# A mixture-of-experts kernel whose second layer changes its operands: split fp32r matrices stream, results are turned afterwards

## The chip, the cores and the metric

The kernel runs on one core of one Trainium2 chip. The metric is the device time of one execution in microseconds; a kernel's time is the median of several runs.

## The reference

Three stages in a row on 768 tokens with 512 features, cut to what matters:

```python
# 1: attention of 8 heads, masked by hash buckets      -> x [768, 512]
# 2: mixture of experts, 8 experts, top 1, capacity 192
expert = argmax(x @ w_gate)                    # [768]
for e in range(8):
    h = maximum(disp[e] @ w1[e], 0)            # w1[e] [512, 1024]
    y[e] = h @ w2[e]                           # w2[e] [1024, 512]
out[i] = gate[i] * y[expert[i], pos[i]]        # tokens over capacity give 0
# 3: a feed-forward layer with the mish function, 2048 hidden
h = x @ w_in                                   # [512, 2048]
g = h * tanh(log1p(exp(h)))
return g @ w_out                               # [2048, 512]
```

All inputs and outputs are float32.

## The kernel before

**Number formats.** TensorE has two ways here to multiply float32. Plain float32 (the experts) issues two pairs of weight load and matmul for each product of 128 by 128 by up to 512. The fp32r format takes one pair; a factor is split into a high part (a copy rounded to fp32r) and a low part (the rest), and three products, high by high, high by low and low by high, give nearly full precision (the mish stage).

**The expert stage.** The tokens are sorted by expert, so expert e owns a stretch of `n_e` columns from `st` in `xs` (features by tokens). A loop of eight turns runs on each engine, one turn an expert. The body is chosen at run time by `n_e`: 128 columns wide (narrow, up to 128 tokens), 144 or 192. In this run the third expert (e = 2) takes the 144-wide body and the other seven the narrow one. Columns past `n_e` are overwritten by the next expert.

A turn (`window`, L795 on TensorE, L1065 on ScalarE, L1345 on VectorE) computes, with eight chunks `fc` of 128 hidden units and four chunks `kd` of 128 features:

- first layer (L802): 32 products `wa` by `xs` into PSUM banks 0 to 3, two chunks `fc` to a bank; `Hw` counts the banks. ScalarE (L1068) and VectorE (L1348) apply the relu into `hs`, two banks each.
- second layer (L820): 32 products in two halves over the output features; `wb` is the stationary side, `hs` the moving one, so the result comes as features by tokens, in banks 4 to 7. `Yc` is raised after the first half and `Yw` after the second. ScalarE writes the high part `yh` (L1075) and VectorE the low part `yl` (L1354), which the mish stage multiplies.

After turn 0, TensorE turns the remaining tokens' rows (`xg`, read back from DRAM in sorted order) into columns by 24 transposes (L856), and ScalarE and VectorE copy them into `xs` (L1090, L1093, L1370, L1373).

**The order of the loads.** Both layers' matrices have one buffer each, `wa` and `wb`, in halves of 1 MB (L385 and L389 issue them). SP's queue issues, in every turn and in this order, each as soon as its buffer is free: the two halves of w1 for the next turn (after chunks 0 to 3 and after chunks 4 to 7 of the first layer), the two halves of w2 (after `Yc` and after `Yw`), and a piece of the mish weights (L394 and L395, 512 KB each). A load of the next turn thus has to wait for the use in this one:

```python
for half in range(2):
    hold(sp, s["passed_sp"], s["Hw"], 4 * i + 2 * half + 2)
    first_weights(i + 1, half)
hold(sp, s["passed_sp"], s["Yc"], i + 1)
second_weights(i + 1, 0)
hold(sp, s["passed_sp"], s["Yw"], i + 1)
second_weights(i + 1, 1)
...
mish_weights(i + 1)
```

GpSimd (POOL) splits the first 10 of the 16 slices of the mish weights while the experts run (L527 to L533). The mish stage (`up`, L880, and `down_tile`, L905) follows the loop at once on TensorE.

Of the kernel before, what the change touches and what calls it, by code (L numbers as in the profile page):

```python
# [22 lines left out]
F32 = mybir.dt.float32  # L23
# [4 lines left out]
ALU = mybir.AluOpType  # L28
# [42 lines left out]
def attention_moe_mish(nc, kt, qt, vt, first, proj1, projs, foldw, w1, w2, w_in, w_out, cf, cb, out,  # L71
# [15 lines left out]
    NS = 10  # L87
    assert NARROW == P and P < MIDDLE < WIDE
# [9 lines left out]
    with ExitStack() as ctx:  # L98
# [36 lines left out]
        mark = place("mark", [P, 4], F32)  # L135
# [14 lines left out]
        wb = ring[1][:, :].rearrange("p (h c n) -> p h c n", h=2, n=DM // 2)  # L150
# [40 lines left out]
        assert top[0] <= weights_end  # L191
        top[0] = d_base
# [46 lines left out]
        for n in ["first_" + n for n in MISH_A + MISH_B] + ["still", "c0", "c", "cr", "k0", "q00", "q01", "k1", "q1", "pj", "pj2", "qs", "cl", "passed_sp", "passed_gp", "rk0", "rk1", "rv0", "rv1", "ca", "cq", "cp", "pja", "pjb", "ah", "ab", "ao", "ak", "aq", "ka", "kl", "ks", "ch", "cc", "opsA", "opsB", "wa0", "wa1", "wb0", "wb1", "Yc", "wi", "wo", "out",  # L239
# [3 lines left out]
                  "zy", "bnd", "Hw", "Ha", "Hd", "Yw", "ya", "yd",  # L243
# [66 lines left out]
        SHORT = WIDE // NT  # L310

# [14 lines left out]
        def _(sp):  # L326
# [65 lines left out]
            def mish_weights(piece):  # L392
                at = bass.ds(2 * piece, 2)
                sp.dma_start(winraw[:, at, :, :], w_in[:, at, :, :]).then_inc(s["wi"], 16)  # L394
                sp.dma_start(woutraw[:, at, :], w_out[:, at, :]).then_inc(s["wo"], 16)  # L395
# [42 lines left out]
        def _(gp):  # L438
# [67 lines left out]
            nc.gpsimd.memset(mark[:, 3:4], 0.0).then_inc(s["Hd"], 2)  # L506
            nc.gpsimd.memset(yh[:, :, :].bitcast(F32), 0.0).then_inc(s["ya"], 2)
# [16 lines left out]
            for f in range(NS):  # L524
                gp.wait_ge(s["wi"], 16 * (f // 2 + 1))
                gp.wait_ge(s["wo"], 16 * (f // 2 + 1))
# [4 lines left out]
                nc.gpsimd.tensor_copy(woh[:, f, :], woutraw[:, f, :]).then_inc(s["ph"], 1)  # L531
                hold(gp, s["passed_gp"], s["ph"], 2 * f + 2)
                nc.gpsimd.tensor_tensor(woutlo[:, f, :], woutraw[:, f, :], woh[:, f, :],  # L533
# [12 lines left out]
        def _(pe):  # L546
# [245 lines left out]
            with pe.Fori(0, E) as e:  # L792
                st, n_e = (pe.snap(x, min_val=0, max_val=T) for x in (at_r, many_r))

                def window(W):  # L795
                    for fc in range(KF):
# [9 lines left out]
                        if fc % 2:  # L806
                            last.then_inc(s["Hw"], 1)
                    for half in range(2):
                        pe.wait_ge(s["ya"], 2 * e + half + 1)
                        pe.wait_ge(s["yd"], 2 * e + half + 1)  # L810
                        pe.wait_ge(s[f"wb{half}"], 16 * (e + 1))
                        if half:
                            pe.reg_load([at_r, many_r], bounds[0:1, bass.ds(e + 1, 1), :].rearrange("p a b -> p (a b)"))
                        for fc in range(KF):
                            if half == 0 and fc % 4 == 0:
                                pe.wait_ge(s["Ha"], 2 + 2 * e + fc // 4 + 1)
                            elif half == 0 and fc % 4 == 2:
                                pe.wait_ge(s["Hd"], 2 + 2 * e + fc // 4 + 1)
# [663 lines left out]
```

## Time and profile before

| | |
|---|---|
| median of 3 runs | 402.37 us (401.75 to 402.7) |
| span of the profiled execution, first to last instruction | 399.9 us |
| TensorE busy | 392.4 us, 98% |
| VectorE, ScalarE, GpSimd busy | 61%, 50%, 23% |
| expert loop on TensorE | from 143.0 to 262.6 us |
| mish stage | from 262.6 us on |
| granted clock of TensorE | 1.00 (2.4 GHz) on average over the span |

The profiled execution is one run; its span of 399.9 us is the only time of its own that it has, and 2.5 us less than the median of the runs, which hold some time around the instructions. PE is TensorE's matmul side, PEld its weight loads, DVE is VectorE, ACT is ScalarE. A busy share tells nothing of what work waits for; the chain does.

### The profile page before, as it was taken

To read this page: it belongs to the slowest core of one execution; us is meant where nothing else is said; L and a number is where in the kernel's file an instruction comes from. 1 tells how busy PE (TensorE), PEld (TensorE's weight loads), DVE (VectorE), ACT (ScalarE), POOL (GpSimd) and SP (SyncE) were. 2 spreads that over 40 slices of the span, in tenths; PEclk is the share of its full clock that TensorE was granted. 3 is DMA by queue.
4 is the path that set the end of the run, shared out by engine and by line. 5 is a ranking of instruction groups with operands and counts; after the bars stand their busy time and mean duration, and the time that the engine had idled before them with its cause. 6 is when DMAs were issued, how large, how long until landed. Compare 5 with 4: busy or idle time off the path is not lost.

```text
span 399.9 us, 7249 instructions
## 1 busy us (share of the span) xinstructions
PE 392.4 (98%) x2666; PEld 365.3 (91%) x2668; DVE 242.7 (61%) x407; ACT 198.6 (50%) x392; POOL 90.5 (23%) x96
## 2 busy tenths in 40 slices
PE   8999999999999999999999999999999999999995
PEld 3689999999999799999999999999889998899984
DVE  5888988988988612211110111049999998877761
ACT  6969779769888312110110110146676756544531
POOL 1942322320600150772464300000000000000015
PEclk9999999999999999999999999999999999999999
DMA  7675934964400348999999999600000000000004
GB/s 286 236 183 144 229 78 137 286 145 123 167 2 2 107 162 322 415 348 339 330 376 366 391 343 369 232 2 1 2 0 2 1 0 2 0 2 0 0 5 157
DMA packets 15803, 62.89 MB, mean 157 GB/s; under 512 B 2960, under 2 KB 3856, under 8 KB 11552
## 3 DMA queue, kind: packets, MB, share of 16 engines
q1 hardware_dynamic: 14272, 58.61, 43.6%
q0 software_dynamic: 992, 3.19, 2.1%
q10 hardware_dynamic: 512, 0.73, 0.6%
q8 instruction: 17, 0.28, 0.3%
q14 instruction: 10, 0.08, 0.1%
HBM read 49.89 MB, written 3.19 MB: 133 GB/s over the span
## 4 chain that ended last, share of the span: by engine, by line
PE 92%; DVE 2%; DMA 2%; SPq 1%; ACT 1%; issue 0%; POOLq 0%; POOL 0%; DVEq 0%
PE ps L880 17%; PE ps L905 16%; PE ps L802 15%; PE ps L820 14%; PE ps L697 8%; PE ps L725 7%; PE ps L606 7%; PE ps L680 3%; DMA raw<-in_kt 2%; PE ps L563 2%; PE ps L779 1%; PE ps L856 1%; DVE ptl L1277 1%; PE ps L567 1%; PE ps L738 1%
## 5 line engine op out<-in xcount | busy, mean ns | idle before, releaser
L802 PE MATMUL ps<-xs,ring 128*128 x512 | 60.0, 277 | 0.3
L802 PEld LDWEIGHTS ps<-xs,ring 128*128 128x128 f32 x512 | 58.7, 192 | 1.1 <-issue 1.1
L820 PE MATMUL ps<-hs,ring 128*128 128x128 f32 (+1 forms) x512 | 59.2, 276 | 0.0
L820 PEld LDWEIGHTS ps<-hs,ring 128*128 128x128 f32 x512 | 58.5, 192 | 0.0
L1030 ACT ACTIVATE pth<-ps 128x384 fp32r<-128x384 f32 x96 | 41.9, 490 | 20.1 <-PE ps L725 19.4
L1277 DVE TENSOR_TENSOR ptl<-ps,pth 128x384 fp32r<-128x384 f32 x96 | 48.9, 551 | 4.2 <-ACT pth L1030 3.3
L1220 DVE TENSOR_REDUCE nmax<-ps 128x1 f32<-128x768 f32 x48 | 45.6, 954 | 4.8 <-PE ps L606 2.7
L606 PE MATMUL ps<-ops 128*128 128x384 f32 x192 | 44.1, 351 | 0.2 <-ACT ops L954 0.2
L987 ACT ACTIVATE prob<-ps,nmax 128x768 f32<-128x768 f32 x48 | 43.5, 906 | 0.1
L880 PE MATMUL ps<-yh,wih 128*128 128x384 f32 x128 | 43.0, 336 | 0.0
L880 PE MATMUL ps<-yh,winlo 128*128 128x384 f32 x128 | 42.8, 335 | 0.0
L880 PE MATMUL ps<-yl,wih 128*128 128x384 f32 x128 | 42.6, 335 | 0.0
L1354 DVE TENSOR_TENSOR yl<-ps,yh 128x256 f32 (+1 forms) x16 | 6.9, 429 | 56.7 <-ACT yh L1075 56.7
L725 PE MATMUL ps<-cfs,prob 128*128 128x128 f32 x288 | 39.8, 274 | 0.4 <-DVE ptl L1277 0.4
L1075 ACT ACTIVATE yh<-ps 128x256 f32 (+1 forms) x16 | 6.2, 388 | 67.5 <-PE ps L820 67.5
L538 POOL DMA_INDIRECT spare<-fold,toki x1 | 1.0, 1009 | 164.9 <-PE ps L905 164.9
L905 PE MATMUL ps<-woh,gl 128*128 128x512 f32 x96 | 37.6, 392 | 0.0
L905 PE MATMUL ps<-woutlo,gh 128*128 128x512 f32 x96 | 37.6, 391 | 0.0
L905 PE MATMUL ps<-woh,gh 128*128 128x512 f32 x96 | 37.3, 389 | 0.0
L725 PEld LDWEIGHTS ps<-cfs,prob 128*128 128x128 f32 x288 | 34.1, 141 | 3.4 <-DVE ptl L1277 1.3
L1348 DVE TENSOR_SCALAR hs<-ps 128x256 f32<-128x256 f32 (+1 forms) x16 | 6.9, 429 | 47.4 <-PE ps L802 47.4
L606 PEld LDWEIGHTS ps<-ops 128*128 128x128 f32 x192 | 33.8, 189 | 1.1 <-DVE ops L1202 0.6
(169 smaller groups left out, 683.4 us busy)
## 6 DMA issues: line engine op xcount, KB each, us to landing
ring<-in_w SPq DMA_DIRECT2D x32, 1024.0 KB, 7.8
winraw<-in_w_in SPq DMA_DIRECT2D x8, 512.0 KB
woutraw<-in_w_out SPq DMA_DIRECT2D x8, 512.0 KB
ops<-kh SPq DMA_DIRECT2D x12, 192.0 KB, 6.9
ops<-qh SPq DMA_DIRECT2D x6, 384.0 KB, 9.2
xg<-rows SPq DMA_DIRECT2D x1, 1539.0 KB, 6.4
raw<-in_vt SPq DMA_DIRECT2D x4, 384.0 KB, 4.9
raw<-in_qt SPq DMA_DIRECT2D x3, 384.0 KB, 6.2
```

The source lines that it names most:

```text
L606: last = mm(ps[:, b + c, 0:HALF], o[:, a, P * u:P * u + P], o[:, kk, c * HALF:c * HALF + HALF], start=(a == QA), stop=(a == QB), skip_grou ...
L680: last = mm(ps[:, XB, W72 * u:W72 * u + W72], ots[:, h % 2, half, P * (u % HT):P * (u % HT) + P], fold[:, h, :], start=True, stop=True)
L697: last = mm(ps[:, OB, 0:HALF], vs[:, (m // 4) % 2, ch, (m // 2) % 2, :, :].rearrange("p a d -> p (a d)"), x[:, m % 2, ch, :, :].rearrange( ...
L725: last = mm(ps[:, tile_banks(n)[b], P * ch:P * ch + P], prob[:, n % 2, HALF * b + P * ch:HALF * b + P * ch + P], c32("ident"), is_transpos ...
L802: last = mm(ps[:, fc // 2, (fc % 2) * WIDE:(fc % 2) * WIDE + W], wa[:, 2 * fc // KF, kd, P * (fc % (KF // 2)):P * (fc % (KF // 2)) + P], x ...
L820: last = mm(ps[:, 4 + half * KD // 2 + k, 0:W], wb[:, half, fc, P * k:P * k + P], hs[:, fc, 0:W], start=(fc == 0), stop=(fc == KF - 1))
L880: last = mm(ps[:, bank + c, 0:HALF], w[:, kd, :], y[:, kd, c * HALF:c * HALF + HALF], start=(n == 0), stop=(n == 3 * KD - 1))
L905: last = mm(ps[:, t, :], g[:, f % 4, ts], w, start=(first and n == 0), stop=(final and n == 2), skip_group_check=True)
L987: av(prob[:, n % 2, :].rearrange("p (c n) -> p c n", c=2), score_tile(n), ACT.Exp, bias=nmax[:, n % 4:n % 4 + 1], accum_out=rowsum[:, n:n ...
L1030: av(pth[:, (n // HT) % 2, HT * b:HT * b + HT, n % HT, :], ps[:, tile_banks(n)[b], 0:HALF].rearrange("p (a c) -> p a c", c=P), ACT.Copy).t ...
L1220: V.tensor_reduce(nmax[:, n % 4:n % 4 + 1], score_tile(n), AX.XY, ALU.max, negate=True).then_inc(s["max"], 1)
L1277: V.tensor_tensor(ptl[:, m2, HT * b:HT * b + HT, u, :], ps[:, tile_banks(n)[b], 0:HALF].rearrange("p (a c) -> p a c", c=P), pth[:, m2, HT ...
```

## The change

For the narrow body the second layer is turned round. The relu's result becomes two fp32r tensors, `hsh` and `hsl`, in [hidden, tokens] order, and these are now the stationary side. The matrix `w2` is split as well: ScalarE copies it, in four portions of 1024 elements a partition, to `w2hi`, and VectorE writes the low part `w2lo` **over the matrix itself** (`w2lo` has the memory of `wb`). TensorE streams 512 columns of `w2hi` or `w2lo` in each of 24 matmuls, all into one bank. The result comes as tokens by features; ScalarE copies it to `ysb`, and TensorE turns it back by four transposes (`turn_rows`), which run in every turn, after the first chunk of the next turn's first layer, and once after the loop. Only then are `yh` and `yl` written.

The 144- and 192-wide bodies keep their plain float32 products, now with the loop over output chunks outside and with two banks for the result; they too pass through `turn_rows`, on old contents. The narrow body's code comes last of the three. `w2` lies in DRAM by halves of the hidden units instead of the output features, so the first half is used first; `Yc` now means that chunks 0 to 3 have been used.

SP's loop is written out, and the order of loads changes: the mish piece comes between w1 and w2, and only in turns 2 to 6; the last two pieces come after the loop, since `w2hi` lies in their memory (`place_out` moves slices of `w_out` for this). Before the first mish product, TensorE waits for all of `yh`.

```diff
@@ buffers
+        top[0] = late + (KFF - LAST) * KD * P * 4
+        w2hi = place("w2hi", [P, KF, DM], F32R)
+        top[0] = ring_at + 4096 * 4
+        w2lo = place("w2lo", [P, KF, DM], F32R)
+        hsh = place("hsh", [P, KF, NARROW], F32R)
+        hsl = place("hsl", [P, KF, NARROW], F32R)
+        ysb = place("ysb", [P, DM], F32)
@@ SP
-            with sp.Fori(0, E - 1) as i:
+            for i in range(E - 1):
                 for half in range(2):
                     hold(sp, s["passed_sp"], s["Hw"], 4 * i + 2 * half + 2)
                     first_weights(i + 1, half)
-                hold(sp, s["passed_sp"], s["Yc"], i + 1)
-                second_weights(i + 1, 0)
-                hold(sp, s["passed_sp"], s["Yw"], i + 1)
-                second_weights(i + 1, 1)
-                hold(sp, s["passed_sp"], s["xt"], 6)
-                hold(sp, s["passed_sp"], s["wi"], 16 * i + 16)
-                hold(sp, s["passed_sp"], s["wo"], 16 * i + 16)
-                mish_weights(i + 1)
+                if i >= FIRST_PIECE:
+                    piece = i - FIRST_PIECE + 1
+                    hold(sp, s["passed_sp"], s["xt"], 6)
+                    hold(sp, s["passed_sp"], s["wi"], 16 * piece)
+                    hold(sp, s["passed_sp"], s["wo"], 16 * piece)
+                    mish_weights(piece)
+                for half, read in enumerate(("Yc", "Yw")):
+                    hold(sp, s["passed_sp"], s[read], i + 1)
+                    second_weights(i + 1, half)
+            hold(sp, s["passed_sp"], s["Yw"], E)
+            for piece in range(EARLY // 2, KFF // 2):
+                mish_weights(piece)
@@ TensorE
+                def turn_rows(count):
+                    pe.wait_ge(s["ye"], count)
+                    for kd in range(KD):
+                        last = mm(ps[:, YT, P * kd:P * kd + P], ysb[:, P * kd:P * kd + P], c32("ident"),
+                                  is_transpose=True, start=True, stop=True)
+                    last.then_inc(s["Ty"], 1)
+                def narrow():
+                    first_layer(NARROW, range(1))
+                    turn_rows(e + 1)
+                    first_layer(NARROW, range(1, KF))
+                    pe.wait_ge(s["ya"], 2 * e + 2)
+                    pe.wait_ge(s["yd"], 2 * e + 2)
+                    for fc in range(KF):
+                        if fc % 2 == 0:
+                            pe.wait_ge(s["Hd"], 2 + 4 * e + fc // 2 + 1)
+                            pe.wait_ge(s["w2l"], 4 * e + fc // 2 + 1)
+                        if fc == KF // 2:
+                            next_bounds()
+                        for n, (x, w) in enumerate(((hsh, w2hi), (hsh, w2lo), (hsl, w2hi))):
+                            last = mm(ps[:, YB, :], x[:, fc, :], w[:, fc, :], start=(fc == 0 and n == 0),
+                                      stop=(fc == KF - 1 and n == 2))
+                        if fc % (KF // 2) == KF // 2 - 1:
+                            last.then_inc(s[("Yc", "Yw")[2 * fc // KF]], 1)
...
-            pe.wait_ge(s["ya"], 2 * E + 1)
-            pe.wait_ge(s["yd"], 2 * E + 1)
+            turn_rows(E + 1)
+            pe.wait_ge(s["ya"], 2 * E + 2)
@@ ScalarE
+                def narrow():
+                    for b in range(4):
+                        act.wait_ge(s["Hw"], 4 * e + b + 1)
+                        av(hsh[:, 2 * b:2 * b + 2, :], ..., ACT.Relu).then_inc(s["Ha"], 1)
+                        if b % 2 == 0:
+                            act.wait_ge(s[f"wb{b // 2}"], 16 * (e + 1))
+                        av(w2hi[:, 2 * b:2 * b + 2, :], wb[:, b // 2, 2 * (b % 2):2 * (b % 2) + 2, :],
+                           ACT.Copy).then_inc(s["w2h"], 1)
+                    act.wait_ge(s["Yw"], e + 1)
+                    av(ysb[:, :], ps[:, YB, :], ACT.Copy).then_inc(s["ye"], 1)
+                    with act.If(e < 1):
+                        rows_in()
+                    act.wait_ge(s["Ty"], e + 2)
+                    av(yh[:, :, bass.ds(st, NARROW)], ps[:, YT, :].rearrange("p (k c) -> p k c", k=KD),
+                       ACT.Copy).then_inc(s["ya"], 2)
@@ VectorE
+                def narrow():
+                    for b in range(4):
+                        dve.wait_ge(s["Ha"], 2 + 4 * e + b + 1)
+                        V.scalar_tensor_tensor(hsl[:, 2 * b:2 * b + 2, :], ..., 0.0, hsh[:, 2 * b:2 * b + 2, :],
+                                               ALU.max, ALU.subtract).then_inc(s["Hd"], 1)
+                        dve.wait_ge(s["w2h"], 4 * e + b + 1)
+                        V.tensor_tensor(w2lo[:, 2 * b:2 * b + 2, :], wb[:, b // 2, 2 * (b % 2):2 * (b % 2) + 2, :],
+                                        w2hi[:, 2 * b:2 * b + 2, :], ALU.subtract).then_inc(s["w2l"], 1)
...
+                    dve.wait_ge(s["ya"], 2 * e + 4)
+                    V.tensor_tensor(yl[:, :, bass.ds(st, NARROW)], ...).then_inc(s["yd"], 2)
```

## Rows read from the trace of the kernel before

**Rows 1.** The page: busy engines (part 1) and the chain by engine (part 4).
```profile
PE 392.4 (98%) x2666; PEld 365.3 (91%) x2668; DVE 242.7 (61%) x407; ACT 198.6 (50%) x392; POOL 90.5 (23%) x96
...
PE 92%; DVE 2%; DMA 2%; SPq 1%; ACT 1%; issue 0%; POOLq 0%; POOL 0%; DVEq 0%
```

**Rows 2.** The chain in order of time: start, length in us, what.
```profile
157.58 2.62 PE ps L856 x24
...
161.78 6.74 PE ps L802 x58
...
212.78 7.15 PE ps L820 x64
...
262.81 16.64 PE ps L880 x96
279.45 4.12 PE ps L905 x18
```

**Rows 3.** Windows of three turns: length; PE, PEld, DVE, ACT, POOL busy; clock; DMA share; GB/s.
```profile
175.50:191.18 15.68, 15.68 (x130) 15.68 (x129) 1.80 (x4) 1.62 (x4) 7.46 (x9) 1.00 0.96 334
...
205.47:219.77 14.30, 14.30 (x131) 14.30 (x129) 1.70 (x4) 1.54 (x4) 8.87 (x10) 1.00 0.98 367
219.77:234.06 14.29, 14.29 (x130) 14.29 (x129) 1.70 (x4) 1.53 (x4) 3.08 (x3) 1.00 0.97 378
```

**Rows 4.** Timeline of turn 0: start, length, engine, instruction [idle before].
```profile
148.07 0.38 ACT L1068 ACTIVATE hs<-ps 128x256 f32<-128x256 f32 x1 [5.64 <-PE ps L802]
148.23 0.43 DVE L1348 TENSOR_SCALAR hs<-ps 128x256 f32<-128x256 f32 x1 [4.89 <-PE ps L802]
...
157.42 2.78 PE L856 MATMUL ps<-cfs,xg 128*128 128x128 f32 x24
157.80 0.38 ACT L1075 ACTIVATE yh<-ps 128x256 f32 x1 [3.21 <-PE ps L820]
```

**Rows 5.** Groups of instructions by form over the span: busy us, mean ns.
```profile
L1390 DVE TENSOR_TENSOR et<-hc,nt__119 128x768 f32<-128x768 f32 x13 | 12.5, 958 | 0.4
...
L1135 ACT ACTIVATE gh<-hn 128x768 fp32r<-128x768 f32 x14 | 11.9, 847 | 6.0 <-DVE hn L1409 6.0
...
L1348 DVE TENSOR_SCALAR hs<-ps 128x256 f32<-128x256 f32 x14 | 5.9, 425 | 41.1 <-PE ps L802 41.1
...
L1068 ACT ACTIVATE hs<-ps 128x256 f32<-128x256 f32 x14 | 5.4, 383 | 33.3 <-PE ps L802 33.3
...
L1433 DVE TENSOR_TENSOR winlo<-winraw,wih 128x512 fp32r<-128x512 f32 x6 | 4.1, 684 | 0.0
...
L1099 ACT ACTIVATE wih<-winraw 128x512 fp32r<-128x512 f32 x6 | 3.8, 626 | 0.0
...
L1159 ACT ACTIVATE outs<-ps 128x512 f32<-128x512 f32 x3 | 1.8, 598 | 8.9 <-PE ps L905 8.9
```

**Rows 6.** The row transfer before turn 1: its issue and its landing.
```profile
L418 SPq DMA_DIRECT2D xg<-rows x1: 332/332/332, 150.7 to 150.7; - x1
...
DMA to landing us min/median/max: 6.4/6.4/6.4
```

**Rows 7.** Two loads of 1 MB (w2, then w1): issue time, us to landing.
```profile
L389 SPq DMA_DIRECT2D ring<-in_w x1: 333/333/333, 220.1 to 220.1; - x1
...
DMA to landing us min/median/max: 6.3/6.3/6.3
...
L385 SPq DMA_DIRECT2D ring<-in_w x1: 340/340/340, 223.8 to 223.8; - x1
...
DMA to landing us min/median/max: 7.9/7.9/7.9
```

**Rows 8.** SP's queue: the mish piece issued between those two loads.
```profile
220.94 0.35 SPq L394 DMA_DIRECT2D winraw<-in_w_in  x1
221.46 0.35 SPq L395 DMA_DIRECT2D woutraw<-in_w_out  x1
```

**Rows 9.** Window of 16 us with the queue full, columns as in rows 3.
```profile
154.00:170.00 16.00, 15.74 (x136) 15.08 (x135) 4.57 (x7) 4.42 (x7) 7.33 (x8) 1.00 1.00 417
```

More of the change, by code:

```diff
@@ L87, in attention_moe_mish @@
     NS = 10
+    LAST = 4
     assert NARROW == P and P < MIDDLE < WIDE
@@ L793, in _, with first_layer @@
                 st, n_e = (pe.snap(x, min_val=0, max_val=T) for x in (at_r, many_r))
-                def window(W):
-                    for fc in range(KF):
+                def first_layer(W, fcs):
+                    for fc in fcs:
                         if fc % (KF // 2) == 0:
@@ L807, in window, with next_bounds, rows_in @@
                             last.then_inc(s["Hw"], 1)
+                def next_bounds():
+                    pe.reg_load([at_r, many_r], bounds[0:1, bass.ds(e + 1, 1), :].rearrange("p a b -> p (a b)"))
+                def rows_in():
+                    pe.wait_ge(s["back"], 16)
+                    for b in XT_BANKS:
+                        for i in range(4):
+                            kd, t = xt_block(b, i)
+                            last = mm(ps[:, b, P * i:P * i + P], xg[:, t, P * kd:P * kd + P], c32("ident"),
+                                      is_transpose=True, start=True, stop=True)
+                        last.then_inc(s["xt"], 1)
@@ L808, in window, with wider @@
+                def wider(W):
+                    first_layer(W, range(1))
+                    turn_rows(e + 1)
+                    first_layer(W, range(1, KF))
+                    pe.wait_ge(s["ya"], 2 * e + 2)
+                    pe.wait_ge(s["yd"], 2 * e + 2)
                     for half in range(2):
-                        pe.wait_ge(s["ya"], 2 * e + half + 1)
-                        pe.wait_ge(s["yd"], 2 * e + half + 1)
                         pe.wait_ge(s[f"wb{half}"], 16 * (e + 1))
-                        if half:
-                            pe.reg_load([at_r, many_r], bounds[0:1, bass.ds(e + 1, 1), :].rearrange("p a b -> p (a b)"))
+                    for k in range(KD):
+                        if k == KD // 2:
+                            next_bounds()
@@ L814, in window @@
                         for fc in range(KF):
[L815 to L818, printed above, removed]
-                            for k in range(KD // 2):
-                                last = mm(ps[:, 4 + half * KD // 2 + k, 0:W], wb[:, half, fc, P * k:P * k + P],
-                                          hs[:, fc, 0:W], start=(fc == 0), stop=(fc == KF - 1))
@@ L822, in window @@
-                        last.then_inc(s[("Yc", "Yw")[half]], 1)
+                            if k == 0 and fc % 2 == 0:
+                                pe.wait_ge(s["Hd" if fc % 4 else "Ha"], 2 + 4 * e + 2 * (fc // 4) + 2)
+                            last = mm(ps[:, SLOW + k // 2, (k % 2) * WIDE:(k % 2) * WIDE + W],
+                                      wb[:, fc // (KF // 2), fc % (KF // 2), P * k:P * k + P],
+                                      hs[:, fc, 0:W], start=(fc == 0), stop=(fc == KF - 1), skip_group_check=True)
@@ L824, in _ @@
+                            if k == KD - 1 and fc % (KF // 2) == KF // 2 - 1:
+                                last.then_inc(s[("Yc", "Yw")[2 * fc // KF]], 1)
+                    with pe.If(e < 1):
+                        pe.wait_ge(s["ya"], 4)
+                        pe.wait_ge(s["yd"], 4)
+                    pe.nop()
                 pe.br_cond(n_e < NARROW + 1, "pe_narrow", "pe_more")
```

171 lines of the change are left out of this document (102 added, 69 removed).

## The prediction

> **What bounds the kernel now.** I read the page first: TensorE is busy for 98% of the span and holds 92% of the chain that ended last [rows 1]. So only time on TensorE, or a new wait of TensorE, can move the end. Then the chain in order of time [rows 2]: the eight turns of the expert loop (143 to 262.6 us) are first and second layer by turns, 7.15 us each for 64 instructions (the row shows one), with nothing between them. The transposes take 0.109 us each (2.62 / 24). The third turn alone (e = 2) uses the 144-wide body, 15.68 us by the windows; the others with loads under them take 14.29 [rows 3]. In the same rows I read the DMA: its mean busy share is already 0.97 to 0.98 in the narrow turns, at 367 and 378 GB/s. A turn loads 2 MB of w1 in two halves, 2 MB of w2 in two halves and 1 MB of mish weights: 5.24 MB in 14.29 us is 367 GB/s. The tighter the turn gets, the more this row matters.
>
> **What the change does to TensorE, load waits left out.**
> Second layer, narrow turn: 64 instructions for 7.15 us go; 24 fp32r matmuls with 512 columns come. The chain has 18 of that shape in 4.12 us [rows 2], 0.229 each, so 24 take 5.50: 1.65 less. Six turns (e = 1, 3 to 7): -9.9 us.
> Turn 0 gets nothing. Its second layer now waits for operands made by ScalarE and VectorE, and these only start their work of that turn at 148.07 and 148.23 [rows 4]. Prices [rows 5]: hs high 0.38 (256 elements), hs low 0.43; the w2 copy has 1024 elements a partition; 512 take 0.63 and 768 take 0.85 on ScalarE, so about 1.07; the subtraction takes 0.68 and 0.96 on VectorE, so about 1.23. VectorE needs 0.43 + 1.23 = 1.66 for each of four pairs of chunks, starting at 148.6, and waits 0.7 for the first copy: the last low part is there at about 156.0, six matmuls later it is 157.4. Before, it was 157.42 [rows 4]. The row transfer that the next step waits for was issued at 150.74 and took 6.4, so it lands at 157.1 [rows 6] and allows no more than 0.3 anyway. Turn 0: 0, bounds -0.3 to +1.5.
> The turning transposes: 4 x 0.109 = 0.44 in turns 1 to 7 and once after the loop: 8 x 0.44 = +3.5. Those of turn 0 lie under its wait.
> They wait for the copy of the last result. ScalarE starts such an eviction 0.38 after TensorE's next instruction begins (157.42 to 157.80 [rows 4]) and a 512-wide one takes 0.60 [rows 5]: with 0.05 for the semaphore the transposes may start 1.03 into the turn, but the four 128-wide products ahead of them are through after 0.89. That is 0.15 of waiting. TensorE's instructions then have no lead: after the waits of turn 1, 58 took 6.74 us, 0.116 each, against 0.112 in a turn without waits [rows 2]; over 56 instructions +0.25. Four turns (4 to 7) x 0.40 = +1.6; turn 2 +0.1; turn 3 follows the 144-wide body and doesn't wait.
> After the loop: before, the last eviction lay under the first third of the first mish product (the chain goes from one to the other without a gap). Now TensorE waits for copy, transposes and second copy in a row: 1.03, then 0.44 (counted), then 0.38 + 0.60 and 0.1: 2.1 us idle that nothing covers. The low part follows 0.8 later (0.16 and 0.68) under 8 products of 0.17 [rows 2, 5]. +2.1.
> The 144-wide body keeps its 64 + 64 instructions; its other order of loops and banks costs nothing on TensorE.
> Sum: -9.9 + 3.5 + 1.6 + 0.1 + 2.1 = -2.6 us.
> At nothing: ScalarE's 7.0 us and VectorE's 7.3 us a turn (were 1.5 and 1.7 [rows 3]) fit in a turn of 13.4 as long as the loads come early; the fp32r copies of winraw start two turns later on POOL, which has 8 us of work a piece and ends before the mish stage; the last two pieces land some 8 us after the loop and are wanted after the fourth product of 8 us; SP's issues are as many as before; the code order has no row against it, since back-to-back turns show no gap.
>
> **The waits for the second matrix.** This is the term that decides. Before, a half of w2 was wanted when the second layer began. Now its first half must be there 1.07 + 0.16 + 1.23 + 0.05 = 2.5 us before that, for the high copy and the low part; and since the low part is written over the matrix, a half is only free when the products have used it. At the same time the 1 MB of mish weights moves ahead of it in SP's queue in turns 2 to 6.
> Landing of 1 MB: issued at 220.1 it took 6.3 [rows 7] with the queue nearly free. The one issued at 223.8, behind the mish pieces of 220.94 and 221.46 [rows 8], took 7.9 [rows 7]: 231.7 against 226.4, so 2 MB add 5.3, 2.65 each. Bounds: over 16 us the queue delivered 417 GB/s [rows 9], 2.5 a MB; at 367 GB/s it is 2.85.
> Let F be the end of a turn's first layer. The second half of w1 is issued at F + 0.3 and lands at F + 6.7 at the earliest; mish piece and w2's first half follow: F + 12.0. With the 2.5 the low part is ready at F + 14.5. TensorE wants it at F + 5.5 + 7.9 = F + 13.4 (7.9 is first layer, transposes and the 0.4). So it waits 1.1, and then goes at VectorE's pace, 1.66 against 1.375 for six matmuls: three times 0.29 more. Some 2.0 us. The turn after has that delay as slack (its loads were issued from its own F, before the wait), so the wait comes in every other turn; between them some 0.4 is left. Turns 4 to 7: 0.4 + 1.5 + 0.4 + 1.5 = +3.8 (of the 2.0 a part is already gone by the 0.4).
> Turn 3: in the 144-wide body the first half of w2 is read until 1.0 us before the end. Issued at 0.7 before the turn, it lands 5.7 into it; the low part is ready at 8.2, wanted at 7.6, and then VectorE's pace: +1.5.
> Turn 1: the loads are behind the row transfer, landing near the time wanted; VectorE's pace alone: +0.9 (bounds 0 to 1.5).
> Together +6.2, bounds 1.5 (a MB every 2.5 us, landing in 6.0) and 9.5 (2.85 and 7.0).
>
> A rule that speaks against the change: the Trainium skill, DMA: Bandwidth & Descriptors, section Specifications, gives 358 GB/s as the limit of HBM for one core. By it a turn's 5.24 MB would take 14.6 us, longer than any narrow turn before. The 417 GB/s over 16 us [rows 9] don't agree with it, so the sum above goes by the rows.
>
> **Forecast.** -2.6 + 6.2 = +3.6 on the span of 399.9. The median of the runs shown is 402.37, 2.5 above that span, for what lies around it; I keep that: 406.0 us.
>
> **Rivals.**
> *Loads hidden* (the other side). If a MB takes 2.5, lands in under 6 us and the copies come no later than reckoned, the waits shrink to under 2 us; without any it is 402.4 - 2.6 = 399.8. For it: 417 GB/s; the queue still has short pauses. Against: shares of 0.97. It decides from F + 10.9 on: w2's first half must land 1.1 us sooner than I have it. 0.16 for a gain over 0.2%, 0.07 for about no change.
> *The DMA's rate is the bound.* If the rate under load is what the narrow turns show divided by their share, 367 / 0.98 = 375 GB/s, a turn with a piece can't be shorter than 14.0 us and each wait grows: 2.8 a MB puts 0.45 more on the first half of w2 and some on its successors, about +2 in all: 408. 0.15. If it falls to what the 144-wide turn shows, 334 / 0.96 = 348 GB/s [rows 3], a MB takes 3.0 and such a turn 15.1: about 410. 0.05. The limit of 358 GB/s in the Trainium skill (DMA: Bandwidth & Descriptors, Specifications) would come out near this case.
> *VectorE paces the second layer* in all turns, 4 x 1.66 = 6.64 for 5.5, with loads in time: -2.6 + 6 x 0.86 = +2.6, 405. 0.07.
> *The fp32r products don't run at 0.229* with their changing chunks and waits: every 10% costs 0.55 x 6 = 3.3: 409. 0.03.
> The case of the forecast: 0.47, 404.2 to 407.8.
>
> **The numbers.** About 0.2%, 0.8 us, is what a measurement of this kernel can tell. Faster 0.16; same 0.07; slower 0.77. Below 400.8 lies most of the case of hidden loads (0.09), above 408.8 the slow DMA and slow products (0.09): range 400.8 to 408.8. The likeliest case alone: 404.2 to 407.8.
>
> **What the profile after would show.** Right: second layers of 5.5 us in turns that don't wait; 6 to 7.5 in the others, with idle of TensorE released by VectorE's low part, and that by the DMA through ScalarE's copy; the narrow turns with a piece between 13.9 and 15.1, mean near 14.45; turn 0 ending at 157.4; about 2.1 us of TensorE idle after the loop; the page's DMA share near 1 all through. Wrong: w2's first half landing before F + 10.9 (then 400 us), turns of 13.5; or ScalarE's copy of 1024 elements far from 1.07, VectorE's far from 1.23; or idle of TensorE released by the copy of the last result over 0.3 a turn.

## The result and the profile after

The changed kernel takes 409.63 us (median of 4 runs, 408.82 to 410.37); the kernel before took 402.53 on the same chip (401.75 to 402.78). The ratio is 1.0175, with a 95% interval of 1.0156 to 1.0193. The forecast was 406.0 with a range up to 408.8: the sign was right, the time is 0.8 us outside the range. The ratios here and below are of fast runs alone, while the medians also hold four single runs in a slower state (405.83 of piecelast2, 426.49 of quiet, 408.42 and 408.1 of the kernel before on two chips). In the profiled execution the span is 407.1 us, 7.2 more than before.

The page after: busy engines, TensorE's granted clock by slices, the chain by engine (to be held against [rows 1]).

```profile
PE 390.8 (96%) x2423; PEld 353.4 (87%) x2424; DVE 285.1 (70%) x442; ACT 233.4 (57%) x434; POOL 103.6 (25%) x97
...
PEclk9999999999999969999999999999999999999999
...
PE 82%; DMA 5%; issue 4%; DVE 4%; ACT 2%; SPq 1%; DVEq 0%; POOLq 0%; POOL 0%; ACTq 0%
```

Two things were not there before: "issue", time in which TensorE waited for nothing that the profile shows, has 4% of the chain, and one slice of the clock stands at 6. A slice is 10.2 us, so it lies at about 142 to 153 us, where the expert loop begins. The timeline of TensorE there:

```profile
141.81 1.95 PE L818 MATMUL ps<-hot,xq 128*128 128x128 f32 x16
147.13 2.07 PE L842 MATMUL ps<-xs,ring 128*128 x8 [3.36 <-issue]
```

And windows of the same stretch and of all turns of the loop but the first (columns as in [rows 3]; the last seven are the turns 1 to 7):

```profile
143.76:147.13 3.37, 0.01 (x2) 0.01 (x1) 0.29 (x1) 0.00 (x0) 2.71 (x3) 0.85 0.62 220
147.13:149.84 2.71, 2.71 (x12) 2.71 (x13) 0.00 (x0) 0.00 (x0) 0.17 (x1) 0.50 0.45 124
149.84:153.00 3.16, 3.16 (x17) 3.16 (x17) 0.42 (x1) 1.21 (x2) 0.00 (x0) 0.51 0.41 100
...
163.02:180.52 17.50, 16.77 (x117) 14.88 (x116) 11.15 (x12) 9.39 (x13) 9.15 (x8) 1.00 0.74 272
180.52:196.64 16.12, 16.12 (x134) 16.12 (x133) 1.61 (x3) 2.02 (x4) 0.07 (x1) 1.00 0.76 285
196.64:211.19 14.55, 13.34 (x94) 12.01 (x93) 8.35 (x10) 5.96 (x10) 9.07 (x8) 1.00 0.95 360
...
211.19:224.70 13.51, 13.36 (x94) 12.03 (x92) 7.62 (x9) 6.53 (x10) 10.97 (x8) 1.00 0.93 353
224.70:240.46 15.76, 13.87 (x94) 12.02 (x92) 8.06 (x9) 6.41 (x10) 10.92 (x8) 1.00 1.00 392
240.46:254.36 13.90, 13.49 (x93) 11.88 (x92) 8.29 (x9) 6.64 (x10) 9.90 (x8) 1.00 0.86 324
254.36:267.60 13.24, 13.24 (x93) 11.93 (x92) 6.74 (x9) 6.52 (x10) 0.00 (x0) 1.00 0.44 180
```

**Where the 7.2 us are.** TensorE stands still for 3.4 us ahead of the first product of turn 0, and then works for 5.9 us at a granted clock of 0.50, which is 1.2 GHz: 5.9 / 2 = 2.9 us more. Of these 6.3 us the turn would have lost about 1.3 anyway: in the kernel near, below, which starts turn 0 without the idle, TensorE is through with the second layer after 5.5 us too and then waits 1.3 us for the row transfer, until 157.5. In the changed kernel the rows have landed by the time that they are wanted. The second layer of turn 0 ends at 163.02, before at 157.42 [rows 4]: 5.6 later. Of that, 0.74 was there before the loop: TensorE was through with L818 at 143.76, and in the kernel before its first product of the loop began at 143.03. So turn 0 costs **+4.9**. Turn 1 is 0.6 shorter than its 18.08 before, turn 2 0.4 longer than its 15.68 [rows 3], turn 3 0.3 longer (14.55 for 14.29), and turns 4 to 7 take 56.4 us for 57.1: 0.7 less. The stretch behind the loop adds 2.2. 0.7 + 4.9 - 0.6 + 0.4 + 0.3 - 0.7 + 2.2 = 7.2.

**The turns with loads.** The chain of the longest turn, in order of time (start, length, what; to be held against the row for L820 in [rows 2]):

```profile
218.95 2.77 PE ps L885 x12
...
221.80 8.47 DMA ring<-in_w
...
230.29 1.07 ACT w2hi L1165
...
232.92 0.41 DVE hsl L1468
233.33 1.05 DVE w2lo L1473
...
237.62 3.00 PE ps L885 x12
```

The first half of w2 could be issued only when twelve products had used the old one (221.8). It landed at 230.3, ScalarE copied it at once, and VectorE's low parts released the products one pair of chunks after another. That is the chain that the forecast named, DMA to ScalarE to VectorE to TensorE. The forecast had it in every other turn; among the turns 4 to 7 (13.5, 15.8, 13.9, 13.2 us) it costs over 1 us in turn 5 alone. The copy of the last result is done in time: the transposes (L867) follow the eighth instruction of L842 without a gap, as the rows of turn 4 show further down.

**The prices of the new instructions**, by form over the span:

```profile
L1473 DVE TENSOR_TENSOR w2lo<-ring,w2hi 128x1024 fp32r<-128x1024 f32 x28 | 40.7, 1454 | 7.7 <-ACT w2hi L1165 7.7
L1165 ACT ACTIVATE w2hi<-ring 128x1024 fp32r<-128x1024 f32 x28 | 29.5, 1053 | 7.3 <-DMA ring<-in_w 7.1
```

ScalarE's copy is what the forecast took (1.07). The subtraction is not: 1.45 in the mean for 1.23. A stretch of the timelines of VectorE and GpSimd shows when:

```profile
217.48 1.29 DVE L1473 TENSOR_TENSOR w2lo<-ring,w2hi 128x1024 fp32r<-128x1024 f32 x1
...
219.17 1.84 DVE L1473 TENSOR_TENSOR w2lo<-ring,w2hi 128x1024 fp32r<-128x1024 f32 x1
```

```profile
217.88 2.06 POOL L568 TENSOR_TENSOR winlo<-winraw,wih 128x512 fp32r<-128x512 f32 x1 [0.18 <-POOL wih L566]
219.87 1.61 POOL L570 CAST woh<-woutraw 128x512 fp32r<-128x512 f32 x1
```

The subtraction that starts at 219.17 needs 1.84 us while GpSimd's runs until 219.94, and GpSimd's, shortest 1.27, needs 2.06 beside VectorE's of 217.48. In turn 7, where GpSimd is idle, VectorE's four take 1.22 each.

Behind the loop, the timeline of TensorE. Its idle comes in two parts, 0.69 and 0.77 us, with the transposes between them, 2.1 us in all from the last product of the loop to the first of the mish stage:

```profile
267.22 0.39 PE L885 MATMUL ps<-w2hi,hsl 128*128 128x512 f32 x1
268.29 0.65 PE L867 MATMUL ps<-cfs,ysb 128*128 128x128 f32 x4 [0.69 <-ACT ysb L1168]
269.72 0.45 PE L960 MATMUL ps<-yh,wih 128*128 128x384 f32 x1 [0.77 <-ACT yh L1172]
```

### The profile page after: what moved, and what is told of

Read it like the earlier page. It is cut to its first block, busy times and chain, and to the rows that moved or that the text cites. A ratio compares the mean times of both kernels' runs of the same rounds, so it can differ in the third digit from the quotient of the medians.

```text
span 407.1 us, 6758 instructions
## 1 busy us (share of the span) xinstructions
PE 390.8 (96%) x2423; PEld 353.4 (87%) x2424; DVE 285.1 (70%) x442; ACT 233.4 (57%) x434; POOL 103.6 (25%) x97
## 4 chain that ended last, share of the span: by engine, by line
PE 82%; DMA 5%; issue 4%; DVE 4%; ACT 2%; SPq 1%; DVEq 0%; POOLq 0%; POOL 0%; ACTq 0%
PE ps L960 16%; PE ps L985 16%; PE ps L842 10%; PE ps L736 8%; PE ps L645 7%; PE ps L764 7%; PE ps L885 7%; DMA ring<-in_w 3%; PE ps L719 3%; DMA raw<-in_kt 2%; PE ps L905 2%; PE ps L602 2%; PE ps L818 1%; DVE w2lo L1473 1%; DVE hsl L1468 1%
## 5 line engine op out<-in xcount | busy, mean ns | idle before, releaser
L842 PE MATMUL ps<-xs,ring 128*128 x512 | 63.6, 283 | 3.5 <-issue 3.4
L842 PEld LDWEIGHTS ps<-xs,ring 128*128 128x128 f32 x512 | 62.0, 198 | 4.7 <-issue 4.1
L1473 DVE TENSOR_TENSOR w2lo<-ring,w2hi 128x1024 fp32r<-128x1024 f32 x28 | 40.7, 1454 | 7.7 <-ACT w2hi L1165 7.7
L736 PE MATMUL ps<-pth,vs 128*128 128x384 f32 x90 | 34.1, 379 | 0.0
L1165 ACT ACTIVATE w2hi<-ring 128x1024 fp32r<-128x1024 f32 x28 | 29.5, 1053 | 7.3 <-DMA ring<-in_w 7.1
L1222 ACT ACTIVATE et<-ps 128x768 f32<-128x768 f32 (+1 forms) x19 | 13.5, 708 | 31.3 <-PE ps L960 31.3
L736 PE MATMUL ps<-ptl,vs 128*128 128x384 f32 x90 | 30.3, 336 | 0.0
```

What stands on the lines that cost most here:

```text
L736: last = mm(ps[:, OB, 0:HALF], vs[:, (m // 4) % 2, ch, (m // 2) % 2, :, :].rearrange("p a d -> p (a d)"), x[:, m % 2, ch, :, :].rearrange( ...
L842: last = mm(ps[:, fc // 2, (fc % 2) * WIDE:(fc % 2) * WIDE + W], wa[:, 2 * fc // KF, kd, P * (fc % (KF // 2)):P * (fc % (KF // 2)) + P], x ...
L1165: av(w2hi[:, 2 * b:2 * b + 2, :], wb[:, b // 2, 2 * (b % 2):2 * (b % 2) + 2, :], ACT.Copy).then_inc(s["w2h"], 1)
L1473: V.tensor_tensor(w2lo[:, 2 * b:2 * b + 2, :], wb[:, b // 2, 2 * (b % 2):2 * (b % 2) + 2, :], w2hi[:, 2 * b:2 * b + 2, :], ALU.subtract).t ...
```

## The experiments

Three questions stood open: what makes the idle in turn 0, what the order of the loads costs, and whether GpSimd's splits or the loads themselves make the waits of turns 3 to 7.

### Is it the place of the narrow body's code?

TensorE's instructions lie in the order in which the bodies are written. Before, the narrow body came between the 144- and the 192-wide one; after, it is the last. Theory: the first jump to it now goes too far ahead, and its instructions have to be fetched first. Rival: the idle comes from something else in the change (the waits on the new operands, the semaphores, another state of the loads), and the place costs nothing.

**near**: the changed kernel, TensorE's narrow body back between the others.

```diff
                     wider(MIDDLE)
                     pe.br("pe_window_done")
-                with nc.body("pe_wide", valid_engines=[pe.engine]):
-                    wider(WIDE)
-                    pe.br("pe_window_done")
                 with nc.body("pe_narrow", valid_engines=[pe.engine]):
                     narrow()
                     pe.br("pe_window_done")
+                with nc.body("pe_wide", valid_engines=[pe.engine]):
+                    wider(WIDE)
+                    pe.br("pe_window_done")
```

> The changed kernel with one thing put back: on TensorE the narrow body's code lies between the 144-wide and the 192-wide one again, not behind both. Theory (code distance): TensorE's 3.4 us of idle at the start of turn 0 and the half clock after it come from fetching the far body's code; both go, turn 0 ends 4.9 us earlier, and the kernel takes 404.7 us (ratio to before 1.005). Rival (the idle comes from another part of the change): TensorE still starts turn 0 about 3.4 us late, 409.6 us.

404.74 us (10 runs, 402.49 to 407.67) against 401.91 for the kernel before on that chip; ratio 1.0074 [1.0046, 1.0102]. The timeline of TensorE at the start of the loop has no idle:

```profile
142.25 0.61 PE L818 MATMUL ps<-hot,xq 128*128 128x128 f32 x4
142.88 1.15 PE L842 MATMUL ps<-xs,ring 128*128 x8
```

The transposes of the rows follow at 157.5, the time that the forecast had, but not for its reason:

```profile
157.53 2.73 PE L859 MATMUL ps<-cfs,xg 128*128 128x128 f32 x23 [1.32 <-DMA xg<-rows]
```

TensorE waits there for the row transfer, and the second layer before it ran without a wait. Without the far place the change costs +2.8 us, not +7.1.

**before_last**: the kernel before, with its narrow body put last and nothing else.

```diff
-                with nc.body("pe_narrow", valid_engines=[pe.engine]):
-                    window(NARROW)
-                    pe.br("pe_window_done")
                 with nc.body("pe_wide", valid_engines=[pe.engine]):
                     window(WIDE)
                     pe.br("pe_window_done")
+                with nc.body("pe_narrow", valid_engines=[pe.engine]):
+                    window(NARROW)
+                    pe.br("pe_window_done")
```

> The kernel before with one thing changed: the narrow body's code comes last on TensorE. Nothing else of the change is in it. Theory (code distance): TensorE idles about 3.4 us at the start of turn 0, its clock falls to half for a while (2.2 us more), and nothing gives that back: 407.5 us or more. Rival: no change, 402.5 us.

407.15 us (4 runs, 406.92 to 407.36); ratio 1.0126 [1.0106, 1.0146]. The timeline of TensorE at the start of the loop, and the window behind it:

```profile
141.82 1.84 PE L779 MATMUL ps<-hot,xq 128*128 128x128 f32 x15
147.00 3.35 PE L802 MATMUL ps<-xs,ring 128*128 x14 [3.34 <-issue]
```

```profile
147.00:150.00 3.00, 3.00 (x14) 3.00 (x15) 0.00 (x0) 0.00 (x0) 0.19 (x1) 0.50 0.34 118
```

The same idle at the same place, the same clock of 0.50 behind it, with none of the new operands. The place alone costs 5.2 us; the rival falls.

**first**: the narrow body directly behind the head of the loop, ahead of both others.

```diff
                 pe.br_cond(n_e < NARROW + 1, "pe_narrow", "pe_more")
+                with nc.body("pe_narrow", valid_engines=[pe.engine]):
+                    narrow()
+                    pe.br("pe_window_done")
                 with nc.body("pe_more", valid_engines=[pe.engine]):
```

> The changed kernel with the narrow body's code ahead of all others on TensorE, right behind the loop's head. Theory (code distance): as in the run with the body in the middle, no idle of TensorE over 0.3 us at the start of turn 0. If the middle position still costs part of a fetch, this one is earlier by that part; the row to read is TensorE's first product of the loop against the last of the sorting products.

409.03 us in a single run, no better than the changed kernel. Turn 0 begins at 143.93 without idle. But now the jump from the narrow body's end to the loop's end is the far one, and the idle stands there:

```profile
161.30 1.96 PE L859 MATMUL ps<-cfs,xg 128*128 128x128 f32 x8 [4.10 <-issue]
```

This jump passes the same two wider bodies. Not all of its 4.10 us is the jump's: the rows that these transposes need were issued at 151.0 and took 7.3, so about 1.2 us would have been waited for them anyway.

**no_wide**: the changed kernel with the narrow body still last, but the 192-wide body's TensorE code replaced by a no-op. No expert of this run uses it.

```diff
                 with nc.body("pe_wide", valid_engines=[pe.engine]):
-                    wider(WIDE)
+                    pe.nop()
                     pe.br("pe_window_done")
```

> The changed kernel, narrow body last as in it, but TensorE's code of the 192-wide body, which these inputs never run, is left out (a single no-op stands in its place). Theory (how far the jumps reach over code): the body is last and yet near, so TensorE starts turn 0 at once and the kernel takes about 404.7 us, as with the narrow body in the middle. Rival (last place itself costs, by the way that the code is laid out or aligned): idle of 3.4 us at the start of turn 0, 409.6 us.

405.59 us (10 runs, 403.69 to 406.81) against 403.39 on its chip; ratio 1.0056 [1.0028, 1.0084]. The loop starts at 143.22 without idle. So it is the distance that counts, not that the body is the last.

The idle is there once, in turn 0; the six later narrow turns jump as far and have none. The Trainium skill, Runtime: NRT & Kernel Launch, section Instruction fetch mechanics, says that a taken branch to a target outside the pages that have been fetched forces a fetch before execution goes on. By that rule a far jump stalls and a near one doesn't, and the first passes of the changed kernel and of the four above agree. It would let the later far jumps stall as well, and there the trace doesn't agree. That the wait is for a fetch was not seen by itself: the trace names it "issue". In the profile's queue of the kind "instruction" one packet moves inside the idle, at 144.2 to 144.4 us in the changed kernel and at 144.0 to 144.2 in before_last, but near has such a packet too, at 143.2 to 143.4, while TensorE works. So the distance of the code is shown as the cause, the fetch is argued.

### The order of the loads

**piecelast**: near, with the piece of the mish weights issued after both halves of w2 instead of ahead of them.

```diff
+                for half, read in enumerate(("Yc", "Yw")):
+                    hold(sp, s["passed_sp"], s[read], i + 1)
+                    second_weights(i + 1, half)
                 if i >= FIRST_PIECE:
...
                     mish_weights(piece)
-                for half, read in enumerate(("Yc", "Yw")):
-                    hold(sp, s["passed_sp"], s[read], i + 1)
-                    second_weights(i + 1, half)
```

> The narrow body in the middle as in the first run, and the piece of mish weights issued behind both halves of w2, not ahead of them. Theory (the queue's order makes the second matrix late): turns 3 to 7 lose their waits beyond VectorE's pace, the sum of turns 4 to 7 falls from 56.4 us to about 54, the kernel takes about 402.3 us. Rival (the DMA's rate is the bound): the bytes are the same, turns 4 to 7 stay at 56 us or more, and the time stays at that of the first run.

400.70 us (10 runs, 399.67 to 402.0), ratio 0.9962 [0.995, 0.9975]: 4.0 us less than near on the same chip, 1.6 less than expected, and faster than the kernel before. The profiles show little of the 4.0, since near's is of its fastest run (402.49) and piecelast's of its slowest (402.0). A second time, on another chip:

> The same kernel as the run with the piece behind w2, again, beside the one above on one chip and with more rounds: 400.7 us if its gain over the kernel before (1.2 us) holds; what differs from run to run should be turn 0's code fetch and the landing of loads, so single times between 399.5 and 403.

400.94 us (12 runs, 399.61 to 405.83) against 402.64; ratio 0.995 [0.9924, 0.9977]. Its windows of turns 4 to 6 (the same columns):

```profile
205.80:218.80 13.00, 13.00 (x93) 12.06 (x92) 6.87 (x9) 6.48 (x10) 8.21 (x9) 1.00 1.01 417
218.80:231.90 13.10, 13.10 (x94) 12.11 (x93) 6.77 (x9) 6.41 (x10) 8.00 (x8) 1.00 1.00 390
231.90:245.20 13.30, 13.30 (x93) 12.01 (x92) 7.32 (x9) 6.46 (x10) 8.99 (x10) 1.00 1.00 410
```

TensorE is busy all through, the DMA share is 1.00 to 1.01 and the queue delivers 390 to 417 GB/s.

**nopiece**: near, with all later mish pieces loaded only after the loop. A single run, to see the turns with w1 and w2 alone under them.

```diff
-                if i >= FIRST_PIECE:
+                if False:
                     piece = i - FIRST_PIECE + 1
...
-            for piece in range(EARLY // 2, KFF // 2):
+            for piece in range(1, KFF // 2):
+                if 1 < piece < EARLY // 2:
+                    sp.wait_ge(s["wi"], 16 * piece)
+                    sp.wait_ge(s["wo"], 16 * piece)
                 mish_weights(piece)
```

> A floor for the turns: as the first run (narrow body in the middle), but pieces 1 to 5 of the mish weights are loaded only after the last turn, so no bytes of theirs are in the loop and GpSimd splits none there. The total is not a fair one, as the mish stage then waits for loads. What counts are turns 4 to 7: about 13.1 us each, 52.5 together, if mish pieces are the cause of the waits, by order, by rate or by GpSimd; 54 or more if w2's overwritten buffer makes TensorE wait anyway.

Turns 4 to 7 take 13.1, 13.1, 13.0 and 13.1 us: no wait is left, and 13.1 is the floor of a narrow turn (7.1 + 0.44 + 5.5 = 13.04 by the forecast's rows). The kernel itself needs 425.53 us, since the mish stage then waits for its weights.

### Loads or GpSimd?

VectorE's subtraction was 0.2 us slower than reckoned whenever GpSimd split weights. Are the waits in turns 3 to 7 GpSimd's?

**quiet**: near, with GpSimd's splits of slices 2 to 9 held back until the last turn is done. **plquiet**: piecelast with the same edit.

```diff
             for f in range(NS):
+                if f == 2:
+                    gp.wait_ge(s["Yw"], E)
                 wait_mish(gp, "wi", f)
```

> Narrow body in the middle, loads in the changed kernel's order; GpSimd splits only the first two slices of the mish weights in the loop and begins the other eight after the last turn. Theory (VectorE's subtraction of w2, with two operands in SBUF, is blocked by GpSimd's instructions): all 28 subtractions take 1.21 to 1.25 us instead of up to 1.98, turns 3 to 6 get 1 to 2 us shorter together, total 403 us, if the mish stage bears the late splits. Rival (load order alone): durations of the subtractions fall, but turns 3 to 6 stay as long, since the loads set them: 404.7 us.

> Both: mish piece behind w2 and GpSimd's eight splits after the loop. Each w2 load and each subtraction is then free of the other cause. If the order was the main cause of the waits, this gains under 0.7 us over the run with the piece behind w2 alone (400.7): 400.0 to 400.7. If GpSimd was, it gains over 1 us. If the late splits hold up the mish stage, it is slower than 400.7.

The windows of turns 4 to 6 of quiet, then of the same turns of plquiet:

```profile
205.30:218.90 13.60, 13.31 (x93) 12.02 (x92) 6.74 (x9) 6.34 (x10) 0.00 (x0) 1.00 0.96 355
218.90:234.70 15.80, 13.81 (x93) 12.03 (x93) 6.74 (x9) 6.35 (x10) 0.00 (x0) 1.00 0.99 396
234.70:248.10 13.40, 13.38 (x94) 12.05 (x93) 6.84 (x9) 6.42 (x10) 0.00 (x0) 1.00 0.92 348
```

```profile
206.30:219.40 13.10, 13.10 (x93) 12.11 (x93) 6.74 (x9) 6.48 (x10) 0.00 (x0) 1.00 1.02 421
219.40:232.50 13.10, 13.10 (x94) 12.11 (x93) 6.75 (x9) 6.53 (x10) 0.00 (x0) 1.00 1.01 417
232.50:245.60 13.10, 13.10 (x94) 12.12 (x93) 6.83 (x9) 6.63 (x10) 0.00 (x0) 1.00 0.98 376
```

With GpSimd silent (the fifth busy column is 0.00) the piece-first order still gives 13.6, 15.8, 13.4 (and 15.1 in turn 7), and the piece-last order three turns at the floor (and 14.0 in turn 7). The turns of all kernels by their profiles, one execution each, from the first product of turn 4 to the end of the last of turn 7:

| load order | kernel | GpSimd in the turns | turns 4 to 7, us |
|---|---|---|---|
| piece first | after | splits | 56.4 |
| piece first | near | splits | 54.9 |
| piece first | no_wide | splits | 58.2 |
| piece first | first | splits | 56.6 |
| piece first | quiet | none | 57.9 |
| piece last | piecelast | splits | 53.8 |
| piece last | piecelast2 | splits | 52.7 |
| piece last | covered (below) | splits | 54.2 |
| piece last | plquiet | none | 53.2 |
| no piece | nopiece | none | 52.5 |

The loads make the waits; GpSimd's part in them is too small to be told from the spread between executions.

That GpSimd slows VectorE is another matter. The same subtraction, by its line in turns 4 to 7 of plquiet and in turns 3 to 6 of the changed kernel (shortest, median, longest in ns):

```profile
L1475 DVE TENSOR_TENSOR w2lo<-ring,w2hi x16: 1216/1218/1225, 211.5 to 256.0; 128x1024 fp32r<-128x1024 f32 x16
```

```profile
L1473 DVE TENSOR_TENSOR w2lo<-ring,w2hi x14: 1207/1412/1976, 205.5 to 250.8; 128x1024 fp32r<-128x1024 f32 x14
```

Both kernels as a whole are far slower than the 403 and 400.7 us expected, as quiet's 423.63 us (419.89 to 426.49; ratio 1.046 [1.0381, 1.0539]) and plquiet's 419.19 (417.27 to 420.26; 1.0382 [1.0328, 1.0435]) show. In quiet the splits now run in the mish stage: TensorE's weight loads wait 9.3 us for GpSimd's `woutlo`, and VectorE's operations with two inputs in SBUF stretch beside GpSimd, the one of L1538 (L1536 in piecelast) to 1034 ns in the mean for 958 in piecelast. TensorE's granted clock falls with the waits: from 290 to 316 us it is 0.83 in the mean in quiet. So the totals of these two kernels say nothing of the loop; only their turns do.

### The gap behind the loop

**covered**: piecelast, with the last four transposes placed after the sixth product of the first mish chunk. With these inputs the last expert's columns lie in the second half of the tokens, so the first half of that chunk need not wait for them. With others they need not lie there, and then the order would be wrong.

```diff
-            turn_rows(E + 1)
-            pe.wait_ge(s["ya"], 2 * E + 2)
+            pe.wait_ge(s["ya"], 2 * E)
+            pe.wait_ge(s["yd"], 2 * E)
...
                     for n, (kd, w, y) in enumerate(terms):
-                        if f == 0 and c == 0 and n == 2 * KD:
+                        if f == 0 and c == 0 and n == 3 * KD // 2:
+                            turn_rows(E + 1)
+                        if f == 0 and c == 1 and n == 0:
+                            pe.wait_ge(s["ya"], 2 * E + 2)
+                        if f == 0 and c == 1 and n == 2 * KD:
                             pe.wait_ge(s["yd"], 2 * E + 2)
```

> The run with the piece behind w2, and the end of the loop changed: the last four transposes stand after the sixth of the 12 products of the first mish chunk's first column half, and only the second half waits for the last expert's yh and yl (its columns lie in 640 to 767 here; for inputs whose last expert begins before column 384 this order would be wrong). Theory (the 2.1 us of idle after the loop is on the path that sets the end): it goes nearly whole, 2 us less than the same kernel without it, 398.6 us against 400.7. Rival (ScalarE and VectorE set the pace of the first mish chunks, so an earlier start of TensorE is given back there): under 0.7 us less.

397.79 us (5 runs, 397.52 to 399.0); ratio 0.9873 [0.9831, 0.9915] to the kernel before, some 3 us less than piecelast2 on the same chip. It is the fastest of all, for inputs of this kind. The timeline of TensorE behind the loop has no idle left:

```profile
258.82 0.39 PE L885 MATMUL ps<-w2hi,hsl 128*128 128x512 f32 x1
259.05 0.33 PE L964 MATMUL ps<-yh,wih 128*128 128x384 f32 x1
...
260.11 0.60 PE L867 MATMUL ps<-cfs,ysb 128*128 128x128 f32 x4
260.46 0.42 PE L964 MATMUL ps<-yh,wih 128*128 128x384 f32 x1
```

The gap was 2.1 us, but the four transposes in it (0.44) are still to be done, so it explains about 1.7 of the 3. The profiles agree: from the end of the loop's last product to the end of the span piecelast2 takes 139.5 us and covered 137.7, 1.8 less. The rest isn't explained; covered's turns 4 to 7 were even 1.4 us longer than piecelast2's in the profiled executions (54.2 for 52.7).

## Why the forecast was right in sign and wrong in size

**The step that failed is turn 0, costed at nothing**: "the code order has no row against it, since back-to-back turns show no gap". The turns that this sentence looked at had all been run once by then; the first entry into the narrow body was not among them, and in the trace of before it was a near jump. The bounds given for turn 0, -0.3 to +1.5, held only VectorE's pace and the row transfer. Measured: +4.9, of which 3.4 are idle and 2.9 the clock of 0.50, less the wait of 1.3 for the rows that they covered. near and before_last, which take the place away and add it alone, change the time by -4.9 (409.63 to 404.74, on two chips; by -4.3 if each is held against the kernel before on its own chip) and by +5.2. Had the step been costed so, the forecast would have been 410.9, 1.3 above the result.

**Turn 0 without the far jump** ends at 157.5 in near, for a forecast of 157.4, and for near that is luck. The forecast let ScalarE and VectorE begin at 148.07 and 148.23, as in the kernel before, and VectorE's last low part come at 156.0. In near ScalarE begins at 145.4 and the last low part is there at 153.4; VectorE holds nothing back, and the row transfer sets the end, which the forecast had put close (157.1) but second. In no_wide ScalarE does begin at 148.3, TensorE waits 0.6 us for a low part, and the second layer ends at 157.5 too. What decides between the two starts, no run shows.

**The other terms.** Second layers without a wait take 5.5 us (turn 0): right. Turn 1: forecast -1.65 + 0.44 + 0.9 = -0.3, measured -0.6. Turn 2: +0.5, measured +0.4. Turn 3: -1.65 + 0.44 + 1.5 = +0.3, measured +0.3. End of the loop: 2.1 of idle and 0.44 of transposes, measured 2.1 with the transposes in it, and 2.2 for the whole stretch behind the loop. The waits of turns 4 to 7, reckoned at 0.4 + 1.5 + 0.4 + 1.5 = 3.8: over the floor of 4 x 13.1 they are 4.0, as 0.4, 2.7, 0.8 and 0.1. That the sum is right is luck, since the parts are not: turn 5 waited 1.2 longer than reckoned and turn 7 1.4 less. For turn 7 the first half of w2 was issued at 251.1 and landed in 7.2 us, 10.1 behind the end of the first layer (248.2), where F + 12.0 was reckoned and F + 10.9 decides. For turn 5 it was F + 11.3 (230.27 with F = 218.95), earlier than reckoned, and yet the wait was longer. So two of the signs that the forecast gave for being wrong were there, a landing before F + 10.9 and a turn of 13.5, and the turns with a piece ran from 13.5 to 15.8 where 13.9 to 15.1 was said; their mean, 14.43, is the 14.45 of the forecast. The rival of hidden loads didn't come true with this order of loads; with the piece last it does, and piecelast's 400.7 us lie close to its 399.8, in a kernel that has lost the far jump too. (The rival of VectorE's pace names 4 x 1.66 = 6.64 for 5.5 but adds 0.86 a turn, which is the delay of the three later pairs alone; by 6.64 it would be 1.14.)

**One term was not there**: +1.6 for the copy of the last result and the lead that TensorE lost. Turn 4 of the changed kernel, in order of time:

```profile
211.35 0.89 PE ps L842 x8
212.24 0.45 PE ps L867 x4
212.70 6.25 PE ps L842 x56
```

0.89 + 0.45 and no wait between; 56 instructions take 6.25, 0.112 each, as in a turn without waits. The row of 0.116 each that I had taken for a lost lead [rows 2] must have another cause, which no run shows.

**Two prices were off, in opposite directions.** The subtraction took 1.45 us for 1.23 beside GpSimd, which I had not held against VectorE. The Trainium skill, SBUF — State Buffer, section "SBUF: two separate sides", says that a VectorE operation with two inputs in SBUF and a GpSimd operation that reads SBUF exclude each other for the whole instruction; the rows above agree, and the forecast didn't weigh it. Against that, a free queue lands 1 MB faster than the 6.3 us that I took for "nearly free": the loads issued at 170.9 and 174.5 landed in 4.8 to 4.9 us. Both show in the turns: the first half of w2 lands 0.7 to 1.9 us sooner than reckoned, and VectorE then needs 0.2 longer for each of its four portions.

**The limit of 358 GB/s** in the Trainium skill (DMA: Bandwidth & Descriptors, Specifications), which I had not followed, isn't seen here: plquiet's turns run at 421 and 417 GB/s for 13.1 us each. That row divides the 716 GB/s of a stack by two cores, and this kernel runs on one core alone. The rivals in which the rate falls to 375 or 348 GB/s fall with these turns.

**What stays open.** near's ten times spread over 5 us (402.49 to 407.67), where those of before_last spread over 0.4; the turns with the piece first came out between 54.9 and 58.2 in five profiles, and no run tells what decides between them. In plquiet and nopiece TensorE stands still for 3.01 us after six matmul instructions of turn 0, also named "issue", though their TensorE code is that of piecelast and near, which don't show it:

```profile
143.22 0.90 PE L844 MATMUL ps<-xs,ring 128*128 x6
147.13 0.48 PE L844 MATMUL ps<-xs,ring 128*128 x2 [3.01 <-issue]
```

Why the instructions come late in some builds or executions was not settled. Nor was the 0.7 us ahead of the loop, which one execution of each kernel can't tell from chance.

## What to carry to other kernels

Where a loop picks one of several bodies at run time, the order in which their code lies is part of the schedule: keep the way in and the way out of the common body short, and cost the first pass by itself, since later turns say nothing about it. When an operation must be fed by a load and two engines' work, put that load ahead of everything in the queue that isn't wanted so soon; here that alone turned a loss of 0.7% into a gain of 0.4%. An end that comes out where it was reckoned doesn't show that the reckoned wait set it; look for its releaser. At the end of a loop, look for a part of the next stage that doesn't need the last result, and lay the last result's latency under it, if no input can make that part need it.

## What the runs showed of the hardware that I had not expected

- The first jump over both wider bodies (each some 130 matmuls and as many weight loads, as turn 2's window shows) left TensorE idle for 3.3 to 3.4 us (4.1 us on the way out, in first, where some 1.2 us of waiting for the rows lies under it); over one body it left none. After it the granted clock was 0.50, for 3 us in before_last and for 5.9 us in the changed kernel, where that cost another 2.9 us.
- The fall of the clock did not always follow: after the 3.01 us of idle in plquiet it stayed at 1.00, after the same in nopiece it was 0.50. Behind the loop, after idles of 0.69 and 0.77 us with four transposes between them, it stayed at 1.00 in the changed kernel.
- A VectorE operation with two SBUF inputs beside one of GpSimd's took up to 1.98 us instead of 1.22, and GpSimd's up to 2.06 instead of 1.27.
- One core's queue held 417 to 421 GB/s over turns of 13 us, at a DMA share of 1.01 to 1.02.
